# Attention scores on the quarters of the array, the value product by key halves, a new token order within fours, and reordered queues

## The reference, cut to what matters

```python
# q, k, v, f_logit: (4, 8, 768, 48)
f = 1.0 / (1.0 + np.exp(-f_logit))
for t in range(S):
    state = f[:, :, t, :, None] * state + np.einsum('bhd,bhe->bhde', k[:, :, t], v[:, :, t])
    y[:, :, t] = np.einsum('bhd,bhde->bhe', q[:, :, t], state)
```

## Time and profile before

| | |
|---|---|
| median of 3 runs | 1233.04 us (1231.67 to 1234.83) |
| profiled execution, first to last instruction | 1221.6 us |
| that execution's time around the span | given for no single execution; the median of the runs lies 11.4 us above the span |
| PE busy | 1185.8 us, 97% |
| DVE busy | 687.1 us, 56% |
| ACT busy | 481.6 us, 39% |
| POOL busy | 479.4 us, 39% |
| DMA | 164.78 MB, mean 135 GB/s |
| attention stage | from the start to about 285 us |

### The profile page before, as it was taken

How to read it: one execution, slowest core, us unless ns; L and a number is a source line. 1 busy time by engine, 2 the same in 40 slices (tenths; PEclk the granted TensorE clock), 3 DMA queues, 4 the chain that set the end, 5 groups by cost and what they waited for, 6 DMA issues and landing times.

```text
span 1221.6 us, 25186 instructions
## 1 busy us (share of the span) xinstructions
PE 1185.8 (97%) x8085; PEld 1037.9 (85%) x8086; DVE 687.1 (56%) x1215; ACT 481.6 (39%) x968; POOL 479.4 (39%) x463
## 2 busy tenths in 40 slices
PE   4999999999999999999999999999999999999998
PEld 4777787788888999999999998888888888888887
DVE  7888988887534454544444554445445454454433
ACT  4666665556333343433333443332322323223212
POOL 8458777754573617163357552220020200100000
PEclk9999999999999999999999999999999999999999
DMA  6233343343577868687788864130030301201000
GB/s 229 72 112 122 123 140 101 109 167 124 188 234 236 250 199 260 202 255 224 237 248 267 248 221 145 52 104 27 28 77 26 104 27 45 60 26 52 27 1 26
DMA packets 109523, 164.78 MB, mean 135 GB/s; under 512 B 48384, under 2 KB 85504, under 8 KB 108928
## 3 DMA queue, kind: packets, MB, share of 16 engines
q1 hardware_dynamic: 97584, 115.48, 30.5%
q0 software_dynamic: 11712, 47.98, 12.6%
q10 hardware_dynamic: 144, 0.20, 0.0%
HBM read 107.45 MB, written 56.16 MB: 134 GB/s over the span
## 4 chain that ended last, share of the span: by engine, by line
PE 82%; POOL 6%; DVE 4%; issue 3%; ACT 2%; DMA 2%; SPq 0%; DVEq 0%; POOLq 0%; ACTq 0%
PE pD L2041 17%; PE pD L2152 12%; PE pA L2152 12%; PE pA L2073 9%; PE pS L2073 9%; PE pA L2180 6%; PE pA L1850 5%; PE pX L2180 3%; PE pS L2180 3%; DVE W L1315 1%; POOL qk L728 1%; POOL fT L709 1%; POOL prods L744 1%; DMA stage<-w 1%; POOL qk L727 1%
## 5 line engine op out<-in xcount | busy, mean ns | idle before, releaser
L2041 PE MATMUL pD<-we,xsH 128*128 x612 | 189.6, 391 | 0.1
L1850 PE MATMUL pA<-W 64*128 64x128 f32 (+3 forms) x1920 | 136.8, 283 | 15.7 <-DVE W L1315 12.2
L1763 DVE TENSOR_TENSOR gs<-pD,sig 128x512 f32<-128x512 f32 x71 | 49.1, 692 | 169.3 <-ACT sig L1229 169.3
L1850 PEld LDWEIGHTS pA<-W 64*128 64x128 f32 (+3 forms) x1920 | 112.7, 170 | 34.8 <-DVE W L1315 18.7
L948 POOL DMA_INDIRECT pair<-y_sorted,y_row x40 | 38.8, 970 | 248.9 <-DMA z_rows<-pair 229.5
L2041 PEld LDWEIGHTS pD<-we,xsH 128*128 128x128 f32 x612 | 114.1, 188 | 22.2 <-issue 0.5
L2041 PE MATMUL pD<-we,xsL 128*128 x306 | 120.1, 392 | 0.0
L1229 ACT ACTIVATE sig<-pD 128x512 f32<-128x512 f32 x71 | 42.6, 600 | 192.4 <-PE pA L2152 192.4
L1315 DVE TENSOR_TENSOR W<-W,prods 128x512 f32<-128x512 f32 (+1 forms) x120 | 101.9, 856 | 22.9 <-PE pA L1850 20.8
L2073 PE MATMUL pA<-we,hidH 128*128 (+1 forms) x448 | 114.5, 336 | 0.0
L1495 DVE STREAM_TRANSPOSE pA<-hidP 128x512 f32<-128x512 f32 x98 | 64.6, 705 | 81.5 <-DMA hidP<-hid_rows 81.3
(11 more groups left out here) (315 smaller groups left out, 2660.9 us busy)
## 6 DMA issues: line engine op xcount, KB each, us to landing
hid_rows<-hid SPq DMA_DIRECT2D x49, 512.0 KB, 3.4
hidP<-hid_rows SPq DMA_DIRECT2D x196, 128.0 KB, 2.9
stage<-w POOLq DMA_DIRECT2D x48, 384.0 KB, 4.7
qk<-qk_t SPq DMA_DIRECT2D x24, 512.0 KB, 3.7
y_sorted<-yo SPq DMA_DIRECT2D x53, 192.0 KB
xs<-x_sorted SPq DMA_DIRECT2D x200, 48.0 KB, 2.1
fT<-f_t SPq DMA_DIRECT2D x12, 512.0 KB, 4.2
vN<-v_n SPq DMA_DIRECT2D x24, 256.0 KB, 2.7
```

Source lines behind the costliest of these rows:

```text
L1763: dve.tensor_tensor(gs[:], pD[:, f % 2 * 512:f % 2 * 512 + TT], sig[f % 2][:], ALU.mult).then_inc(s_u, 1)
L1850: ins = pe.matmul(pA[par][keys, s, c * P:(c + 1) * P], both[r, 1, c, keys], both[r, 0, c], start=True, stop=True)
L2041: ins = pe.matmul(hidden_bank(t, h), (xsL if a else xsH)[t.par][:, k * P:(k + 1) * P], we[:, bass.ds(at + (b * WE + k * F + h * HF), HF)], ...
```

## The change

- Level 0 to 4 scores are computed only within the two halves of a tile (first 64 keys by first 64 queries, last 64 by last 64), each a 64x64 quarter of the array; level 5 only between them (first 64 keys, last 64 queries). PSUM and the masks have 64 columns a head instead of 128, and the masks' lower partitions hold the second half's. `take_masked` copies 64 columns a head.
- The value product is made in two parts: `attend_late` over the last 64 keys for the last 64 queries, `attend` over the first 64 keys for all queries. The inherited state's part is its own function, `inherit`, by 64 columns.
- q, k, v and the noise come with the first two tokens of each four exchanged (`in_turn` on the host, undone on the output). Each block's centre is then its token 0 in the new order, and `to_centres` on DVE decays tokens 1, 2 and 3 in one operation; POOL's `turn_first` is gone. ACT's `decay_factors` has four smaller operations for two.
- The queues of POOL, ACT, DVE and PE are reordered; `merge_inner` runs two pairs ahead instead of one, `scores(., 0)` of the next pair stands at the end of a body, and the splits of the first expert's weights stand later. SP's queue is as it was.

The diff, cut to its core (the other bodies are reordered in the same manner):

```diff
+        def among(k, first, left):
+
+            return first <= k < NP - left
...
+        pool.tensor_copy(v[lower, :, 0:nb // 2], v[lower, :, nb // 2:]).then_inc(done, 1)
...
-                f4, g4 = (in_fours(FG[k % 2][:, :, n]) for n in range(2))
-                pool.tensor_tensor(f4[:, :, :, 0::3], f4[:, :, :, 0::3], f4[:, :, :, 1:3], ALU.mult).then_inc(s_fix, 1)
-                pool.tensor_tensor(g4[:, :, :, 3], g4[:, :, :, 3], g4[:, :, :, 2], ALU.mult).then_inc(s_fix, 1)
-
-            def turn_first(t):
-
-                pool.wait_ge(s_qk[t % 4], 16 * (t // 4 + 1))
-                fg = FG[t // 2 % 2][:, t % 2].rearrange("p a (b u) -> p a b u", u=BASE)
-                v = qk[t % 4].rearrange("p a c (b u) -> p a (c b) u", u=BASE)
-                pool.tensor_tensor(v[:, 0, :, 0], v[:, 0, :, 0], fg[:, 1, :, 1], ALU.mult)
-                pool.tensor_tensor(v[:, 1, :, 0], v[:, 1, :, 0], fg[:, 0, :, 1], ALU.mult).then_inc(s_u0, 1)
+                both = FG[k % 2].rearrange("p t n (b u) -> p t n b u", u=BASE)
+                pool.tensor_tensor(both[:, :, :, :, 3], both[:, :, :, :, 3], both[:, :, :, :, 2],
+                                   ALU.mult).then_inc(s_fix, 1)
+                pool.tensor_tensor(both[:, :, 0, :, 0], both[:, :, 0, :, 0], both[:, :, 1, :, 1],
+                                   ALU.mult).then_inc(s_fix, 1)
 
             def products(k):
 
-                pool.wait_ge(s_fix, 2 * k + 1)
+                pool.wait_ge(s_fix, 2 * k + 2)
...
             def body(k):
-                p, r, s = k - 1, k - 2, k - 3
-                if is_pair(p) and not first_of_sequence(2 * p):
-                    decay_state(2 * p)
-                if is_pair(r) and r < NP - 1:
-                    add_noise(r)
-                if is_pair(k + 2) and k:
-                    clamp(k + 2)
-                if is_pair(k + 1):
-                    merge_inner(k + 1)
-                    turn_first(2 * k + 2)
-                    turn_first(2 * k + 3)
-                    products(k + 1)
-                if k == 0:
-                    clamp(2)
+                s, p, n, u = k - 3, k - 1, k + 1, k + 2
+                if among(u, 2, 0):
+                    clamp(u)
                 if is_pair(p) and not last_of_sequence(2 * p + 1):
                     decay_state(2 * p + 1)
-                if is_pair(s):
+                if among(n, 1, 0):
+                    products(n)
+                if among(s, 0, 2):
                     scatter(s, 0)
-                if is_pair(s):
+                if is_pair(k) and not first_of_sequence(2 * k):
+                    decay_state(2 * k)
+                if among(s, 0, 2):
                     scatter(s, 1)
+                if among(u, 1, 0):
+                    merge_inner(u)
+                if among(p, 0, 1):
+                    add_noise(p)
...
-                act.activation(FG[k % 2][:, :, 0], fs[:], ACT.Exp, scale=-1.0)
-                act.activation(FG[k % 2][:, :, 1], fs[:], ACT.Exp).then_inc(s_fg, 1)
+                both = FG[k % 2].rearrange("p t n (b u) -> p t n b u", u=BASE)
+                part, (tiles, _), (kinds, _), (blocks, n), _ = both.ap
+                first = bass.AP(both.tensor, both.offset, [part, [tiles, 2], [blocks, n], [kinds + 1, 2]])
+                f4 = fs.rearrange("p t (b u) -> p t b u", u=BASE)
+                act.activation(first, f4[:, :, :, 0:2], ACT.Exp, scale=-1.0)
+                act.activation(both[:, :, 0, :, 1], f4[:, :, :, 1], ACT.Exp)
+                act.activation(both[:, :, 0, :, 2:], f4[:, :, :, 2:], ACT.Exp, scale=-1.0)
+                act.activation(both[:, :, 1, :, 2:], f4[:, :, :, 2:], ACT.Exp).then_inc(s_fg, 1)
...
+            def to_centres(t):
+
+                dve.wait_ge(s_fix, 2 * (t // 2) + 1)
+                dve.wait_ge(s_qk[t % 4], 16 * (t // 4 + 1))
+                fg = FG[t // 2 % 2][:, t % 2].rearrange("p a (b u) -> p a b u", u=BASE)[:, :, :, 1:]
+                v = qk[t % 4].rearrange("p a c (b u) -> p a (c b) u", u=BASE)[:, :, :, 1:]
+                dve.tensor_tensor(v, v, fg, ALU.mult).then_inc(s_qkd, 1)
...
+                to = aT[t % 4][:, :, :, 0:HS].rearrange("p a c b -> p (a c) b")
+                fr = pA[t % 2][:, :, 0:HP * HS].rearrange("p a (c b) -> p a c b", b=HS)
                 if n:
                     h = LEVELS[n - 1]
-                    to = aT[t % 4].rearrange("p a c (b s u) -> p a (c b) s u", s=2, u=h)[:, :, :, 1]
-                    fr = pA[t % 2].rearrange("p a (b s u) -> p a b s u", s=2, u=h)[:, :, :, 1]
+                    to = to.rearrange("p m (b s u) -> p m b s u", s=2, u=h)[:, :, :, 1]
+                    fr = fr.rearrange("p a c (b s u) -> p a c b s u", s=2, u=h)[:, :, :, :, 1]
                     at = (n - 1) * HP * HS
-                    mk = mask[:, at:at + HP * HS].rearrange("p (b u) -> p b u", u=h)
-                    mk = mk.unsqueeze(1).to_broadcast([P, 2, HP * HS // h, h])
+                    mk = mask[:, at:at + HP * HS].rearrange("p (c b u) -> p c b u", c=HP, u=h)[:, 0, 0:HS // (2 * h)]
+                    mk = mk.unsqueeze(1).to_broadcast([P, H, HS // (2 * h), h])
                 else:
-                    to = aT[t % 4].rearrange("p a c b -> p (a c) b")
-                    mk = mask[:, len(SMALL) * HP * HS:].unsqueeze(1).to_broadcast([P, H, P])
-                    fr = pA[t % 2].rearrange("p a (c b) -> p (a c) b", b=P)
+                    at = len(SMALL) * HP * HS
+                    mk = mask[:, at:at + HS].unsqueeze(1).to_broadcast([P, H, HS])
...
+                left, right = slice(0, HS), slice(HS, P)
+                blocks = ((left, right),) if n == NL else ((left, left), (right, right))
                 for c in range(HP):
-                    for s in range(2):
-                        r = slice(HS * s, HS * (s + 1))
-                        keys = slice(0, P - LEVELS[n - 1] if n >= MASKED else P)
-                        ins = pe.matmul(pA[par][keys, s, c * P:(c + 1) * P], both[r, 1, c, keys], both[r, 0, c],
-                                        start=True, stop=True)
+                    for keys, asks in blocks:
+                        for s in range(2):
+                            r = slice(HS * s, HS * (s + 1))
+                            ins = pe.matmul(pA[par][keys, s, c * HS:(c + 1) * HS], both[r, 1, c, keys],
+                                            both[r, 0, c, asks], start=True, stop=True)
...
+                if p == NP - 1:
+                    low_weights(0, 0)
+                    low_weights(0, 1)
...
-                if k == NP - 1:
-                    low_weights(0, 0)
...
+            def inherit(t):
 
                 pe.wait_ge(s_upd[t % 2], NL * (t // 2 + 1))
-                pe.wait_ge(s_rect[t % 2], RECTS * (t // 2 + 1))
+                pe.wait_ge(s_yt, t)
+                pe.wait_ge(s_spread, states_up_to(t - 1))
+                for c in range(HP):
+                    for s in range(2):
+                        pe.matmul(pD[HS * s:HS * (s + 1), c * P:(c + 1) * P], stateB[1 - t % 2][:, c, s],
+                                  W[t % 6][:, 0, c], start=c == 0, stop=False, skip_group_check=True)
+
+            def attend_late(t):
+
+                pe.wait_ge(s_rect[t % 2], RECTS * (t // 2) + RECTS - 1)
                 pe.wait_ge(s_v[t % 4], 16 * (t // 4 + 1))
                 if t == 0:
                     pe.wait_ge(s_clear, 1)
                 else:
                     pe.wait_ge(s_yt, t)
-                inherits = not first_of_sequence(t)
-                if inherits:
-                    pe.wait_ge(s_spread, states_up_to(t - 1))
-                if inherits and cs[0] == 0:
-                    for c in range(HP):
-                        pe.matmul(pD[:, c * P:(c + 1) * P], stateB[1 - t % 2][:, c].rearrange("p s d -> p (s d)"),
-                                  W[t % 6][:, 0, c], start=c == 0, stop=False, skip_group_check=True)
-                for c in cs:
-                    y = pD[:, c * P:(c + 1) * P]
+                late = slice(HS, P)
+                for c in range(HP):
                     for s in range(2):
-                        ins = pe.matmul(y[HS * s:HS * (s + 1)], vN[t % 4][:, 2 * c + s], aT[t % 4][:, s, c],
-                                        start=not inherits, stop=True, skip_group_check=True)
-                if cs[-1] == HP - 1:
-                    ins.then_inc(s_y, 1)
+                        ins = pe.matmul(pD[HS * s:HS * (s + 1), c * P + HS:(c + 1) * P], vN[t % 4][late, 2 * c + s],
+                                        aT[t % 4][late, s, c, 0:HS], start=first_of_sequence(t) and c == 0,
+                                        stop=False, skip_group_check=True)
+                ins.then_inc(s_late, 1)
+
+            def attend(t):
+
+                pe.wait_ge(s_rect[t % 2], RECTS * (t // 2 + 1))
+                pe.wait_ge(s_late, t + 1)
+                soon = slice(0, HS)
+                for c in range(HP):
+                    for s in range(2):
```

(52 more changed lines are left out.)

290 lines of the change are left out of this document (126 added, 164 removed).

## The result

The changed kernel has a median of 1217.86 us (1215.81 to 1219.67, four executions) beside 1232.36 us (1231.64 to 1234.83) for the kernel before on the same chip: a ratio of 0.9882, 95% interval 0.9862 to 0.9903. It is 14.5 us faster, where 39.8 were forecast. The time lies inside the range, but under half of the gain came. The profiled execution took 1219.67 us, its span 1218.0.

The account below looks back on a forecast made before the run. PE was taken to bound the attention pairs, with DVE 1.0 us behind. Eleven shorter periods (-38.3), start (-3) and tail (+1.5) gave -39.8 us: 1221.6 - 39.8 + 11.4 = 1193.2 us, range 1180 to 1228.

Parts of the forecast that it names:

- The score level: PE in attention: a level of 32 matmuls, four quarters abreast, takes 0.67 us instead of 1.09 (last level 1.02).
- (b): Score levels on PE: small matmuls have a price each, 1.0 us a level; total 1227 us; chance 0.07.
- (c): Score matmuls on PE go only two abreast, 1.20 us a level; slower, total 1249 us; chance 0.09.
- The value product: PE in attention: key halves and half-wide inherited-state matmuls add 0.58 us a tile, 1.16 us a pair.
- DVE: DVE's work in a pair of token tiles falls from 20.8 to 18.7 us, mean pair 17.9, together about 18.3.
- The new period: Attention pairs: 18.3 us plus 1.1 us idle give 19.4 us instead of 22.88; eleven such periods save 38.3 us.
- Each is costed at nothing: POOL's new order and scatter issues, ACT's extra decay operations and SP's loads in attention add no time.
- Rival (d): PE, less busy, falls to its lower clock in stretches, at twice the time of a level; slower; chance 0.03.
- The start: First pair: without POOL's four first-token decays, merges and DVE's second decay finish earlier; -3 us (bounds -4 and -1).
- The tail: End of attention: DVE's two remainders of the first expert's weights move behind the last scores; +1.5 us (bounds 0 and +3.5).
- The later stages: Experts and feed-forward after attention are untouched, move as one block and keep their length.

Follow-up runs that it names:

- the order alone: Changed kernel with the scores, copies, masks and products of before, keeping the new queue order and the three-token decay: 1208.98 us, ratio 0.9857 to before.
- the best version: Changed kernel with score levels 3 and 4 full width and the inherited state's product in 4 matmuls, scatters in their place: 1184.51 us, ratio 0.9677 to before.
- the quarters alone: Kernel before with quarter scores, half-width copies and masks and the value product by key halves, old order and decays: 1213.63 us, ratio 0.9905 to before.

## Why the prediction was right or wrong

**The score level** was right in kind and a little dear: 0.67 forecast, 0.52 to 0.62 us measured, four quarters abreast. With it fall rivals (b) and (c), and the rule of the Trainium skill ("TensorE: Matmul & The Clock Gate", section "Wait — 56ns, not 53.3ns?") of some 25 ns between starts: 32 matmuls in 0.62 us with the start of the group in it are 19 ns each. The trace does not agree with that rule across quarters.

**The value product** had +0.58 a tile. Fully fed, the early keys take 0.98 us (71.70 to 72.68) and the late ones up to 0.80, of it 0.15 a wait: 1.63 to 1.78 for 1.18, as forecast.

**DVE** had 18.3 us a pair; the fully fed pair has 15.67, with its fewer operations, and a pair without the scatters 102.26 / 6 = 17.0. The masked copies came as priced. The three-token decay, forecast to add 0.8 a pair, adds nothing (999 for 1062 ns), and the doubling fell from 897 to 820 ns. More was taken back from POOL's collisions than the 0.5 that I took; that collisions are the cause remains an argument.

**The new period**, 19.4 us, is the step that failed. PE's 18.1 and DVE's 18.3 were sums of streaming and work. The instructions' own way to PE was in no term, though PE's count per pair went from 294 to 501, and though I wrote of the scatters, "Each is costed at nothing". Where PE was fed, a pair took 16.4 to 18 us; without the scatters 17.9 over six pairs; with them 21.6, though PE's and DVE's work had both been priced too high. The 3.7 us between the last two are 26 us over seven pairs. Rival (d), the lower clock, got 0.03 and the condition "less busy": it was part of the mechanism, as the second step of it.

**The start** had -3 us. The first router product comes at 45.8 us for 54.6 before, 8.8 earlier, of which one shorter pair explains 3.5 to 6: the start gave 3 to 5.

**The tail** had +1.5 us and was the second failure. By the tenth router product the changed kernel is 29.8 us ahead (231.7 and 261.5 us), where the forecast had 3 + 9 x 3.5 = 34.5; by the first expert tile, which starts at 272.8 and 289.5, it is 16.7 ahead, and at the end of the span 3.6. Some 26 us go after the tenth router product, by profiles that are good to 1%. I priced two DVE operations there. What the rows show is PE standing still for 3.49 and 2.68 us, and a mean clock of 0.72 up to the first expert tile and 0.92 in the 92 us after it. The scatters beside these stops aren't what makes them. The kernel without scatters in the loop, in which POOL issues none before 260.63 us, has the same stretch and the same two stops, 2.87 and 2.67 us:

```profile
204.00:243.70 39.70, 33.41 (x639) 28.19 (x636) 21.96 (x55) 20.01 (x52) 3.14 (x9) 0.74 0.29 108
...
213.65 0.48 PE L1869 MATMUL pA<-W 64*64 64x64 f32 x4 [2.87 <-issue]
```

From the tenth router product to the first expert tile it needs 39.7 us, the changed kernel 41.1, the kernel before 28.0, the order alone 34.2 with its own matmuls. The second stop is a wait that the new order made, though the view puts it down to issue:

```profile
258.80 2.85 ACT L1070 CAST we<-stage 128x1536 fp32r<-128x1536 f32 x2
262.15 0.47 ACT L1035 COPY x<-pX 128x384 f32<-128x384 f32 x1
262.73 0.63 PE L1885 MATMUL pX<-ident,W 128*128 128x128 f32 x4 [2.68 <-issue]
```

PE's `turn_keys` may write `pX` only once ACT has copied x out of it, and in ACT's new order both splits of the first expert's weights stand ahead of that copy. The order alone has this stop too (1.54 us); before, these matmuls waited 0.5 us at most, for DVE. This is a step that the forecast left out: it moved DVE's part of the weights, and did not look at what ACT's part holds up. Even the best version, with a full clock in all its pairs, gives back 10 us there, with a clock of 0.85 from 211.8 to 256.3 us. Which part of the tail's loss is the clock, which the stops and which the lost overlap of neighbouring pairs was not tried apart. The later stages were forecast to keep their length. From the first expert tile to the end of the span they take 945.2 us, 932.1 before and 936.2 in the best version; 5.5 us of it are PE idle in the first 92 us, the rest is within the 1% of the profiles, with a clock of 0.99 in the experts' stretch.

**What stays open.** The runs show that the burst of scatters, the number of PE's instructions and the trickle belong together. They don't show through which part of the chip: whether the scatters' descriptors, their issue or their packets hold the stream up. The instruction packets themselves aren't lengthened: between 60 and 265 us those within 0.5 us of a scatter take 1.10 us in the mean, the others 1.03 (1.32 and 1.10 in the kernel before). And there is a second kind of stop, with and without scatters, which the trickle isn't. The 3.49 us end at 241.67, 2.35 us after the start of a packet of instructions at 239.32; the 2.87 us without scatters end at 213.65, 2.35 after one at 211.30. It looks as if PE waits there for a packet that comes late, and why it comes late is open. No kernel was made to hold the clock full with the idle time in place; the kernel without scatters has 1.1 us of idle time a pair at full clock, so not every idle time lowers it.

## What to carry to other kernels

Splitting matmuls over the array's quarters halves their streaming and doubles their instructions; price both, and look at where other queues issue bursts of indirect DMAs, since there PE trickled here. Split only as many levels as bring PE under the next engine: here four of six on quarters, with the inherited product in 4 matmuls (ratio 0.9677), beat all six (0.9882) by 2%. And measure the halves of a change apart: two that give 1.4% and 1.0% gave 1.2% together. The order alone was held by PE's work, the quarters alone by waits for DVE, and together they met a third limit, PE's instructions beside the scatters, that neither met to this extent alone.

## What the runs showed of the hardware that was not expected

- While POOL issued four indirect DMAs in a row, PE was fed four to six matmuls each 0.75 us, in two kernels with different forms of matmul (64 and 128 columns). With 424 matmuls a pair instead of 501 it kept its full pace beside four scatters.
- 32 matmuls of 64x64 with 64 columns took 0.52 to 0.62 us from start to start, and with 128 columns 1.02, where 16 full-width ones took 1.09.
- Alternating 64-wide and 32-wide tiles made 32 matmuls take 2.82 us instead of 1.02, so some 0.22 us for each of the eight changes of width, the one behind the level with them; 64 beside 48 wide cost nothing (the level before it, split that way, stayed at 1.02).
- A few microseconds of a starved PE were followed by levels of nearly twice the length: 1.91 us for 1.10, and 1.99 for 1.10.
- The two longest stops of PE that no engine explains, 3.49 us beside scatters and 2.87 without any, both ended 2.35 us after the start of a packet of instructions.
- A stop put down to issue can be a wait for a buffer: the 2.68 us before 262.73 ended with ACT's copy out of `pX`.
